# Attention, mixture of experts and Fourier mixing in one program: last layers in groups of four tiles, the sequence transform by row tiles, the last expert tile's second layer inside the loop

## The reference

```python
x = attention(q, k, v)                      # 16 heads, local window and block summaries
x = moe(x, w_gate, w_local, w1, w2)         # 8 experts 512 -> 1024 -> 512, one expert per token
X = np.fft.fft(np.fft.fft(x, axis=1), axis=2)
u = x + np.real(X)                          # the sequence transform, then that of the features
un = (u - mean(u)) / np.sqrt(var(u) + 1e-6)
out = u + np.maximum(un @ w_ch1, 0.0) @ w_ch2   # 512 -> 2048 -> 512, the "last layers"
```

## Time and profile before

| | us |
|---|---|
| median of 3 runs | 667.31 |
| the runs | 666.71, 667.31, 671.98 |
| the profiled execution | 672.55 |
| its span, first to last instruction | 670.6 |
| PE busy in it | 625.5 (93%) |
| DVE, ACT, POOL busy | 364.0, 270.8, 129.2 |

### The profile page before, as it was taken

One profiled execution on the slowest core, in us unless ns is written; L12 is line 12 of the kernel. 1 busy time (PEld: TensorE's weight loads), 2 busy tenths in 40 slices (PEclk: granted clock), 3 DMA queues, 4 the chain that ended last, 5 costly groups with the idle time before them and its releaser, 6 DMA issues.

```text
span 670.6 us, 11120 instructions
## 1 busy us (share of the span) xinstructions
PE 625.5 (93%) x3282; PEld 531.4 (79%) x3283; DVE 364.0 (54%) x956; ACT 270.8 (40%) x593; POOL 129.2 (19%) x155
## 2 busy tenths in 40 slices
PE   4799998899889999998899999999999999999993
PEld 3799998878667888886534589988999899989992
DVE  4788687568472585232451666655444544454441
ACT  3488775445132364111011534453443343433330
POOL 5566544203610010010000412030000310000001
PEclk9999999879999999998979999999999999999997
DMA  6958533694454455310503240001000100010001
GB/s 152 170 125 181 127 77 120 216 323 150 183 195 167 157 162 164 152 63 17 203 0 112 92 173 1 0 1 49 1 0 1 47 0 0 0 47 0 0 0 47
DMA packets 59300, 61.61 MB, mean 92 GB/s; under 512 B 42688, under 2 KB 42816, under 8 KB 58240
## 3 DMA queue, kind: packets, MB, share of 16 engines
q1 hardware_dynamic: 54384, 47.21, 24.0%
q0 software_dynamic: 3440, 11.32, 4.5%
q10 hardware_dynamic: 1440, 2.64, 1.3%
HBM read 48.27 MB, written 12.89 MB: 91 GB/s over the span
## 4 chain that ended last, share of the span: by engine, by line
PE 79%; DVE 6%; issue 4%; DMA 3%; ACT 3%; SPq 1%; another core or an unknown queue 1%; POOL 1%; DVEq 0%; ACTq 0%; POOLq 0%
PE bank L2011 20%; PE bank L1998 18%; PE bank L1876 10%; PE bank L1851 9%; PE bank L1713 3%; PE bank L1938 2%; PE bank L1753 2%; PE bank L1722 2%; ACT arena L703 1%; PE bank L1839 1%; PE bank L1951 1%; PE bank L1863 1%; PE bank L1962 1%; PE bank L1736 1%; PE bank L1745 1%
## 5 line engine op out<-in xcount | busy, mean ns | idle before, releaser
L1998 PE MATMUL bank<-parts 128*128 128x384 f32 x768 | 146.1, 338 | 2.1 <-DVE parts L1392 2.1
L2011 PE MATMUL bank<-parts 128*128 128x512 f32 x576 | 143.8, 394 | 0.7 <-DVE parts L1646 0.3
L1392 DVE TENSOR_TENSOR parts<-arena,parts 128x512 fp32r<-128x512 f32 (+1 forms) x140 | 98.8, 737 | 83.0 <-ACT parts L856 77.9
L1998 PEld LDWEIGHTS bank<-parts 128*128 128x128 f32 x768 | 135.5, 188 | 7.1 <-DVE parts L1392 2.8
L2011 PEld LDWEIGHTS bank<-parts 128*128 128x128 f32 x576 | 106.7, 188 | 21.7 <-DVE mid L1614 1.3
L1851 PE MATMUL bank<-parts 128*128 128x512 f32 x312 | 77.8, 403 | 3.1 <-issue 2.3
L1876 PE MATMUL bank<-parts 128*128 128x512 f32 x312 | 76.2, 401 | 4.9 <-DVE parts L1392 4.5
L856 ACT ACTIVATE parts<-arena 128x512 fp32r<-128x512 f32 x64 | 40.4, 631 | 82.2 <-PE bank L2011 82.2
L1876 PEld LDWEIGHTS bank<-parts 128*128 128x128 f32 x312 | 58.8, 192 | 17.9 <-issue 3.6
L1851 PEld LDWEIGHTS bank<-parts 128*128 128x128 f32 x312 | 59.0, 193 | 16.5 <-issue 4.5
L1392 DVE TENSOR_TENSOR parts<-bank,parts 128x512 fp32r<-128x512 f32 (+1 forms) x56 | 35.1, 649 | 33.6 <-ACT parts L846 23.5
(11 more groups left out here) (221 smaller groups left out, 790.0 us busy)
## 6 DMA issues: line engine op xcount, KB each, us to landing
mid<-in_moe_w SPq DMA_DIRECT2D x16, 512.0 KB, 6.8
arena<-in_moe_w SPq DMA_DIRECT2D x16, 512.0 KB, 7.2
arena<-in_moe_w_ch SPq DMA_DIRECT2D x2, 2048.0 KB
arena<-in_moe_w_ch SPq DMA_DIRECT2D x4, 1024.0 KB, 9.2
arena<-in_k SPq DMA_DIRECT2D x16, 192.0 KB, 3.2
arena<-in_q SPq DMA_DIRECT2D x16, 192.0 KB, 4.0
mid<-in_v SPq DMA_DIRECT2D x16, 192.0 KB
x_all<-folded_y SPq DMA_DIRECT2D x6, 512.0 KB, 7.3
```

Of the source, the lines that this page charges most:

```text
L1392: return dve.tensor_tensor(out, whole, upper.bitcast(F32), ALU.subtract)
L1998: last = pe.matmul(bank[2 + f % 2][:, 0:GN], w[:, f % 2, r], x[:, par, c, :], start=(c == 0 and w is m1_hi and x is cT_hi), stop=(c == DC ...
L2011: last = pe.matmul(bank[4 + t][:, :], x[:, f % 2, r], w[:, f % 2, :], start=(f == 0 and x is g_hi and w is m2_hi), stop=(f == MC - 1 and w ...
```

## The change

1. GT = 4 and GROUPS = 3. A step is now 12 matmuls of 512 columns in `first` and 12 of 512 in `second` (four banks), 48 steps instead of 64. `TILES` says which tile stands at which place. The first group has two natural and two mirrored tiles, the second four mirrored ones, the third four natural ones. The loops over groups are written out on PE, ACT and DVE.
2. `finish` takes each tile as soon as its own last matmul is done (`tile_ps`). Stores follow the kind of the rows: SP for natural ones, POOL for mirrored ones. `cen` and `out_sb` no longer share memory.
3. ACT centres four tiles of the first group before the last layers, not three.
4. DVE folds by row tile: even and odd part of a tile together. For batch 0, PE goes by row tile too, for all five outputs.
5. The second layer of the last tile stands in the loop, behind a test whether tile n is the last. 28 matmuls instead of 40 follow.

```diff
-GT = 3
+GT = 4
-TURN_AT = {5: (0,), 7: (1,), 9: (2,), 11: (3,)}
+TURN_AT = {7: (0,), 9: (1,), 11: (2,), 13: (3,)}
+TILES = (0, KC, 1, KC + 1) + (KC + 2, ST + KC, ST + KC + 1, ST + KC + 2) + (2, ST, ST + 1, ST + 2)
...
@@ gpsimd @@
+            for n in MIRRORED:
+                pool.wait_ge(o_sb, n + 1 + GT)
+                pool.indirect_dma_start(out=out_rows, ...
@@ scalar, vector @@
             centre(2)
+            centre(3)
...
             def fold(b):
                 for c in range(KC):
+                    fold_even(b, c)
+                    fold_odd(b, c)
...
             def finish(g):
-                dve.wait_ge(l2_ps, MC * (g + 1) + TWO)
                 for c in range(GT):
                     n = GT * g + c
+                    if c < GT - 1:
+                        dve.wait_ge(tile_ps, (GT - 1) * g + c + 1)
+                    else:
+                        dve.wait_ge(l2_ps, MC * (g + 1) + TWO)
@@ tensor @@
                         turn_hidden(n)
-            second_layer(used - 1)
+                        with pe.If(used < n + 2):
+                            second_layer(n)
...
+                if b == 0:
+                    for j in range(KC):
+                        pe.wait_ge(even_ok, j + 1)
+                        for o, r, free, n, done in to:
+                            cosines(o, r, j)
+                        if j == KC - 1:
+                            pe.wait_ge(row_ok, 1)
+                            for o, r, free, n, done in to:
+                                alternating(o, r).then_inc(done, 1)
+                        pe.wait_ge(odd_ok, j + 1)
+                        for c in range(FD):
+                            last = sines(c, j)
...
-            for _ in range(40):
+            for _ in range(28):
                 pe.matmul(bank[7][:, :], xT_hi[:, 0:P], w1_hi[:, 0, 0:512], start=True, stop=True)
```

More of the change, by code:

```diff
@@ L368, in build, with stored @@
         counts_at = [x[:, BESIDE:BESIDE + (ST + 1) * E].rearrange("p (t e) -> p t e", t=ST + 1) for x in (O_BANK[0], Q_BANK)]
+        def stored(n):
+            kind, signal = (NATURAL, natural_out) if n in NATURAL else (MIRRORED, mirrored_out)
+            return signal[n % GT], 16 * len([m for m in kind if m <= n and m % GT == n % GT])
         block = ctx.enter_context(nc.Block())
@@ L641, in _ @@
             centre(1)
-            pool.wait_ge(ln_ok, GROUPS)
+            pool.wait_ge(ln_ok, 2)
             pool.wait_ge(ct_ps, 2 * DC)
@@ new lines, in _ @@
+            for g in range(GROUPS):
+                for f in range(MC):
+                    F = MC * g + f
+                    more = F + 1 < MC * GROUPS
+                    if more:
+                        lower1(F + 1, (f + 1) % MC)
+                    if F == 0:
+                        add_back(1, 1)
+                        add_back(1, 2)
+                    dve.wait_ge(ghi_ok, F + 1)
+                    dve.scalar_tensor_tensor(g_lo[:, f % 2, :], bank[2 + f % 2][:, 0:GN], 0.0, g_hi[:, f % 2, :].bitcast(F32),
+                                             ALU.max, ALU.subtract).then_inc(glo_ok, 1)
+                    if f == 0 and g:
+                        finish(g - 1)
+                    if f - 1 in TURN_AT and g + 1 < GROUPS:
+                        centred(g + 1, (g + 1) % 2, TURN_AT[f - 1])
+                    if more:
+                        lower2(F + 1, (f + 1) % MC)
+                    if g == 0 and 1 <= f <= NT:
+                        statistics((f - 1) // GT, (f - 1) % GT)
+                        if f % GT == 0:
+                            norm((f - 1) // GT)
+                    if g == 0 and f == INVERT_AT:
+                        invert()
@@ new lines, in along_sequence, with cosines, sines @@
+                to = [(bank[c][:, 0:CW], slice(P * c, P * c + P), yc_sb, FD * b + c + 1, yc_ps) for c in range(FD)]
+                to.append((bank[6][0:1, 0:CW], slice(HD, HD + 1), z_sb, b + 1, z_ps))
+                def cosines(o, r, j):
+                    pe.matmul(o, even[:, b, j, r], cosS[:, j, :], start=(j == 0), stop=False)
+                def sines(c, j):
+                    return pe.matmul(bank[2 + c][:, 0:HS], odd[:, b, j, P * c:P * c + P], sinS[:, j, :], start=(j == 0), stop=(j == KC - 1))
@@ new lines, in alternating @@
+                def alternating(o, r):
+                    return pe.matmul(o, even_row[:, b, r], const("odd", 1), start=False, stop=True)
+                if b == 0:
+                    for o, r, free, n, done in to:
+                        pe.wait_ge(free, n)
+                    for c in range(FD):
+                        pe.wait_ge(ys_sb, c + 1)
+                    for j in range(KC):
+                        pe.wait_ge(even_ok, j + 1)
[3 more added lines that the diff above has]
+                            pe.wait_ge(row_ok, 1)
+                            for o, r, free, n, done in to:
+                                alternating(o, r).then_inc(done, 1)
+                        pe.wait_ge(odd_ok, j + 1)
+                        for c in range(FD):
+                            last = sines(c, j)
+                            if j == KC - 1:
+                                last.then_inc(ys_ps, 1)
+                else:
+                    for o, r, free, n, done in to:
+                        pe.wait_ge(free, n)
+                        for j in range(KC):
+                            pe.wait_ge(even_ok, KC * b + j + 1)
+                            cosines(o, r, j)
+                        pe.wait_ge(row_ok, b + 1)
+                        alternating(o, r).then_inc(done, 1)
+                    for c in range(FD):
+                        pe.wait_ge(ys_sb, FD * b + c + 1)
+                        for j in range(KC):
+                            pe.wait_ge(odd_ok, KC * b + j + 1)
+                            last = sines(c, j)
+                        last.then_inc(ys_ps, 1)
@@ L2012, in second @@
                                          stop=(f == MC - 1 and w is m2_lo))
+                    if f == MC - 1 and t < GT - 1:
+                        last.then_inc(tile_ps, 1)
                 last.then_inc(l2_ps, 1)
-            for _ in range(40):
+            for _ in range(28):
                 pe.matmul(bank[7][:, :], xT_hi[:, 0:P], w1_hi[:, 0, 0:512], start=True, stop=True)
```

241 lines of the change are left out of this document (80 added, 161 removed).

## The result

The changed kernel takes 645.42 us (median of 643.38, 644.01, 646.84 and 647.34). The kernel before, run beside it, took 669.52 (666.71 to 671.98). The ratio is 0.9641, with a 95% interval of 0.9579 to 0.9702: 3.6% faster.

What follows compares the result with a forecast made beforehand. PE was taken as the bound, holding 79% of the chain. From the profiled 672.55 us: last layers -4.6, last expert tile and batch 0 -10.9, start of the last layers +0.7, end -7.1, giving 650.65; range 647.5 to 657.5.

Steps and rivals of the forecast that it cites:

- New: 24 x 0.231 = 5.55 a step: Last layers: 24 matmuls of 512 columns a step, 48 steps, 266.4 us against 268.2; with turns and stops, gain 4.6.
- Time goes by columns, and nearly nothing by matmul: Last layers: 0.458 and 0.451 ns per column at 384 and 512 columns, so fewer matmuls would save little, 1.8 us.
- The last expert tile: Second layer of that tile: starts 1.2 us earlier and loses 1.5 less to half clock, result 2.7 earlier.
- batch 0: Sequence transform of batch 0 on PE: 8.2 us less, 5.1 from the clock and 3.1 from overlap.
- the start of the last layers: Features and first weights: ACT centres a fourth tile first; loss 0.7 us, a third between bounds 0 and 2.0.
- the end: Behind the last matmul: 3.6 us instead of 10.75, with SP's store and drain last; gain 7.1.
- the lower pair: Runs of the kernel before at 666.7 and 667.3 us, taken to lack the half clock that cost 5.1.
- A: Rival, second layer of the last tile and transform: the clock falls all the same, 652.4 to 655.8 us; chance 0.30.
- B: Rival, start of the transform: empty rounds and unread matmuls end two us late, 652.7 us; chance 0.10.
- C: Rival, behind the last matmul: SP's drain is as long as POOL's, gain 3.5, time 654.2 us; chance 0.08.
- E: Rival, last layers: 512-column matmuls of `first` take over 0.231 us; at 0.24, 5.2 more, 655.8; chance 0.08.
- D: Rival, expert tile loop: PE's jumps over the new second layer fetch code; 677.7 us at 6 each; chance 0.02.

Runs made afterwards that it cites:

- rows_only: The kernel before with only the new fold and transform by row tiles, the last tile's second layer staying behind the loop: 664.06 us beside 669.05, ratio 0.9933.
- layer_only: The kernel before with only the last tile's second layer in the loop and 28 unread matmuls: 666.09 us, ratio 0.9984.
- mirrored_last: The changed kernel with the second and third group exchanged, so that POOL stores last: 649.43 us.
- finish_late: The changed kernel with every output of a group waiting for the group's last matmul: 651.0 us.
- after_third: The changed kernel once more, unchanged: 645.51 us.

## Why the prediction missed, point by point

**Last layers: the step that failed.** The step is "New: 24 x 0.231 = 5.55 a step". It prices an unbroken run of 512 columns by nine matmuls that all lie behind a change of width, where the distances had not settled. Settled, a matmul is 0.2267 and a step 5.44, which is 5.3 us less in 48 steps; stops and turns gave 0.5 less than forecast. The gain is 9.4 instead of 4.6. The 4.3 us that 64 steps with changes of width cost stood at nothing in the forecast.

"Time goes by columns, and nearly nothing by matmul" was wrong too, but it hardly moved the number. The two prices per column, 0.458 and 0.451 ns, already differ by most of what the fixed part makes, and the forecast's 268.2 - 266.4 = 1.8 is that difference, against the 2.6 of 192 matmuls fewer. The same numbers set a page against the trace: the Trainium skill, page "TensorE: Matmul & The Clock Gate", section "Back-to-back issue gap", gives an isolated matmul a fixed 2.5 ns beside its columns, and says itself that a stream with weight loads has another spacing. A fixed part there is, but these runs show 13.3 ns, for matmuls that each have a weight load. The prediction threw out the form of the rule together with its number; it should have kept the form and asked which rows could show the size.

**The other terms.** The last expert tile (2.7), batch 0 (8.1 for 8.2), the start of the last layers (0.7) and the end (7.2 for 7.1) came as worked out, and rows_only, layer_only, mirrored_last and finish_late show the mechanisms one by one. Batch 0 came out so near partly by luck: its 8.1 is the distance from a profile with 10.2 us of half clock to one of the five of 14 with none. The loss of a third of the 2.0 at the start was a choice between bounds, and happened to be exact. Upstream, where nothing was changed, the profiles differ by 1.4 us the other way: the same kernel had its last turning at 310.36 in the first profile and at 305.44 in after_third's, with three stretches of half clock ahead of it (17.1 us in all) and with none. Half clock alone does not order these starts: in mirrored_last the last turning is at 304.92, with 13.7 us of it ahead.

In sum: 650.65 - 4.8 for the last layers + 1.4 upstream + 0.1 for small things is the profiled 647.34. The median is 1.9 below that one.

**The median of before.** "I take it that the lower pair had no such stretch" is not borne out: none of the four profiles of that transform was without half clock, though none of them is known to be of the lower pair. Upstream, where the profiles of the changed kernel and its variants lie up to 5.4 us apart, is the likelier source of the pairs; no run shows it. The gain against the median of 667.31 was 21.9, not 16.7, and against the 669.52 measured beside it 24.1.

**Rivals.** A came true in part, at the 1.7 that it gave for a short stretch: none in the first profile, one or two in nine of 14, eight times behind the one-row matmuls, which it did not name, and twice behind the stop ahead of the transform, which it did. B: the queue was 0.89 late behind the layer, with 1.83 to spare before the transform. C and E didn't occur. D: eight jumps more cost nothing that shows; the layer was free at 1.73 behind the turning. **The range** was too narrow below: it let the last layers be better by stops alone, never by the price per matmul, which carried 1,152 matmuls. Rival E asked only whether that price could be higher.

## What to carry to other kernels

A price read from short runs of mixed shapes holds for that mix alone: look for a long run of one shape before you price one. With a step of fixed columns, fewer and wider matmuls of one width save a fixed part each, and a change of width costs about as much as two or three of them (25 to 41 ns against 13.3). At the end of a program count what lies behind the last matmul engine by engine, the drain included, and let the engine with the cheap drain store last.

## What the runs showed of the hardware

- Matmuls of fp32r with 128 rows and columns of weights and a weight load each, in long runs: 120.0, 173.3 and 226.7 ns for 256, 384 and 512 columns, which is columns / 2.4 GHz + 13.3 ns.
- A change of width slows the next five to nine: 41 ns in sum from 384 to 512 columns, 26 from 512 to 384, 28 from 256 to 512, and 25 behind one matmul of 500 among those of 512. It did not slow those of 256 behind 512.
- TensorE's clock fell to 1.2 GHz with PE busy throughout, in a run of 60 records whose weights and moving data had one row; one column of weights left it at 2.4 GHz. Why, no run here shows.
- POOL's drain took 3.59 us in every kernel, at the end or in mid-program; SP's took 7 ns, at either place.
